# The start of an attention and two-layer network kernel: own banks for x, w_lo in parts, other load order, fewer spins

## The reference

```python
for t in range(S):
    kt, vt, rt, wt = (k[:, :, t], v[:, :, t], r[:, :, t], w[:, :, t])
    cur = np.einsum('bhd,bhe->bhde', u[None] * kt, vt)
    y[:, :, t] = np.einsum('bhd,bhde->bhe', rt, state + cur)
    state = wt[:, :, :, None] * state + np.einsum('bhd,bhe->bhde', kt, vt)
# x = y as [3072, 384]
h = x @ w_in;  g = h * np.clip(h + 3.0, 0.0, 6.0) / 6.0;  x = g @ w_out
h = x @ w_in2; g = h * (1.0 / (1.0 + np.exp(-h)));        x = g @ w_out2
```

## Time and profile before

| | us |
|---|---|
| median of three runs | 890.62 (890.15 to 891.52) |
| profiled execution, its own time | 890.26 |
| span in the profile | 888.6 |
| PE busy | 884.1 (99%) |
| DVE, ACT, POOL busy | 477.6, 314.6, 124.5 |

### The profile page before, as it was taken

How to read it: one execution, slowest core, us unless ns; L and a number is a source line. 1 busy time by engine, 2 the same in 40 slices (tenths; PEclk the granted TensorE clock), 3 DMA queues, 4 the chain that set the end, 5 groups by cost and what they waited for, 6 DMA issues and landing times.

```text
span 888.6 us, 14887 instructions
## 1 busy us (share of the span) xinstructions
PE 884.1 (99%) x5608; PEld 733.8 (83%) x5608; DVE 477.6 (54%) x718; ACT 314.6 (35%) x543; POOL 124.5 (14%) x136
## 2 busy tenths in 40 slices
PE   9999999999999999999999999999999999999998
PEld 7888888888888888888888888888888888888897
DVE  9898667747754864776445443342433343342423
ACT  5634233333233333333444543333232333333222
POOL 2133224304322340342000000000000000000000
PEclk9999999999999999999999999999999999999999
DMA  9545323314422431351223000200200200200201
GB/s 275 174 143 166 92 75 105 93 59 107 126 58 71 126 100 62 93 140 24 107 71 107 1 1 1 36 1 1 35 0 0 35 0 0 35 0 0 36 1 36
DMA packets 89874, 57.61 MB, mean 65 GB/s; under 512 B 76144, under 2 KB 77296, under 8 KB 89840
## 3 DMA queue, kind: packets, MB, share of 16 engines
q1 hardware_dynamic: 89840, 57.15, 23.7%
HBM read 47.18 MB, written 9.96 MB: 64 GB/s over the span
## 4 chain that ended last, share of the span: by engine, by line
PE 98%; DVE 1%; DMA 0%; issue 0%; DVEq 0%
PE bank L882 15%; PE bank L884 15%; PE bank L883 15%; PE bank L906 14%; PE bank L908 13%; PE bank L907 13%; PE bank L937 3%; PE bank L964 2%; PE bank L956 2%; PE bank L945 1%; PE bank L920 1%; PE bank L918 1%; PE bank L919 1%; PE bank L969 1%; PE bank L997 1%; DMA unit_in<-w_fm 0%
## 5 line engine op out<-in xcount | busy, mean ns | idle before, releaser
L882 PE MATMUL bank<-x_hi,w_hi 128*128 (+1 forms) x576 | 226.7, 393 | 0.0
L884 PE MATMUL bank<-x_hi,w_lo 128*128 (+1 forms) x576 | 224.4, 390 | 0.0
L883 PE MATMUL bank<-x_lo,w_hi 128*128 (+1 forms) x576 | 224.3, 389 | 0.0
L494 ACT CAST g_hi<-g 128x512 fp32r<-128x512 f32 x192 | 119.3, 621 | 286.4 <-PE bank L908 221.6
L906 PE MATMUL bank<-g_hi,w_hi 128*128 128x512 f32 x528 | 206.1, 390 | 0.0
L908 PE MATMUL bank<-g_hi,w_lo 128*128 128x512 f32 x528 | 205.5, 389 | 0.0
L907 PE MATMUL bank<-g_lo,w_hi 128*128 128x512 f32 x528 | 205.4, 389 | 0.0
L669 DVE TENSOR_TENSOR g<-g,bank 128x512 f32<-128x512 f32 x96 | 66.0, 687 | 226.0 <-ACT g L488 226.0
L676 DVE TENSOR_TENSOR g_lo<-g,g_hi 128x512 fp32r<-128x512 f32 x192 | 144.9, 755 | 4.4 <-ACT g_hi L494 4.4
L882 PEld LDWEIGHTS bank<-x_hi,w_hi 128*128 128x128 f32 x576 | 108.1, 188 | 24.5 <-issue 0.3
L884 PEld LDWEIGHTS bank<-x_hi,w_lo 128*128 128x128 f32 x576 | 108.1, 188 | 22.8
(11 more groups left out here) (102 smaller groups left out, 653.6 us busy)
## 6 DMA issues: line engine op xcount, KB each, us to landing
unit_in<-rkv_tm SPq DMA_DIRECT2D x20, 576.0 KB, 5.8
unit_in<-rk_fm SPq DMA_DIRECT2D x22, 448.0 KB, 4.6
unit_in<-w SPq DMA_DIRECT2D x9, 768.0 KB, 4.3
x<-w SPq DMA_DIRECT2D x7, 768.0 KB, 7.3
unit_in<-w_fm SPq DMA_DIRECT2D x23, 226.2 KB, 5.4
passing<-tmp SPq DMA_DIRECT2D x20, 256.0 KB, 2.0
keys_tok<-passing SPq DMA_DIRECT2D x80, 64.0 KB, 2.5
out<-tmp SPq DMA_DIRECT2D x60, 64.0 KB, 2.2
```

What stands on the lines that cost most here:

```text
L494: nc.scalar.copy(g_hi[:, p, :], g[:, p, :]).then_inc(ghi_done, 1)
L882: nc.tensor.matmul(h_ps[j % 2][:, :], wh, xh, start=k == 0, stop=False)
L883: nc.tensor.matmul(h_ps[j % 2][:, :], wh, xl, start=False, stop=False)
L884: last = nc.tensor.matmul(h_ps[j % 2][:, :], wl, xh, start=False, stop=k == KT - 1)
```

## The change

- Each x gets a bank of its own (banks 4, 3, 2, 5); `first_values` no longer waits for `xlo`, and starts on the even heads' half of the mask. `xlo` of all four units goes behind the last mask on DVE.
- `first_hidden` replaces `hidden` for tiles 0 and 1: hi*hi (waits for `xhi`), then the low weights (waits for one part of `w_lo`), then the low x.
- `w_lo` of chunks 0 and 1 is made in parts of 1, 1, 2 and 1, 3 tiles.
- The first unit's decays are loaded and scanned in two halves; decays and features of the next unit go ahead of the values of the one before.
- Unit 3's own sums come behind unit 1's values; its keys are turned into bank 7.
- Spins: one fewer after unit 0, and the spins before unit 3's own sums, before unit 2's values and before the first tile go.
- ACT: `first_state(3)` before `whi(1)`; `whi(2)` behind the first tile's `gate` and `ghi`. The memset of `v_mid` moves from DVE to POOL.

```diff
-        first_outer, first_keys, first_x, first_sums = bank[2], bank[3], bank[4], bank[7]
-        last_x = first_scores[0][0]
+        first_sums = bank[7]
+        first_outer = [bank[2], bank[2], bank[2], bank[7]]
+        first_keys = [bank[3], bank[3], bank[3], bank[7]]
+        first_x = [bank[4], bank[3], bank[2], bank[5]]
+        Q0_FIRST, Q0_THEN = (0, 1, 3, 6), (4, 9, 7, 10)
+        Q1_FIRST, Q1_THEN = (2, 5, 8, 11), (1, 4, 7, 10)
...
-            first_load(0)
-            first_load(1)
-            first_load(2)
+            first_decays_load(0)
+            first_features_load(0)
+            first_u_load()
+            first_decays_load(1)
+            first_features_load(1)
+            first_values_load(0)
+            first_decays_load(2)
+            first_features_load(2)
+            first_values_load(1)
+            first_decays_load(3)
+            first_features_load(3)
             load_raw(0)
-            first_load(3)
+            first_values_load(2)
+            first_values_load(3)
             load_raw(1)
...
-            xhi(2, 2, 0, first_x)
-            xhi(3, 3, 0, last_x)
+            xhi(2, 2, 0, first_x[2])
+            xhi(3, 3, 0, first_x[3])
+            first_state(3)
             whi(1)
-            first_state(3)
-            whi(2)
             for j in range(2):
                 tile(j, j, ACT.Relu)
+                if j == 0:
+                    whi(2)
                 if j in WHI_SLOTS:
                     whi(WHI_SLOTS[j])
...
             def scan(a, w, loaded, count):
...
+                    dve.wait_ge(half_loaded, 16)
+                    scan_back(w, HALF, PAIRS * SEG).then_inc(half_scanned, 1)
+                    dve.wait_ge(loaded, count)
+                    scan_back(w, 0, HALF).then_inc(back_done, 1)
...
+            wlo_tiles(0, 0, 1, part_done)
+            for b in range(B):
+                xlo(b, b, 0, first_x[b])
+            wlo_tiles(0, 1, 2, part_done)
+            wlo_tiles(0, 2, 4, wlo_done)
+            wlo_tiles(1, 0, 1, part_done)
             gated(0, 0, 1.0, ALU.min)
+            wlo_tiles(1, 1, 4, wlo_done)
             glo(0, 0)
...
             def first_values(b):
-                if 0 < b < B - 1:
-                    pe.wait_ge(xlo_done, b)
+                v, scores, x_bank = firsts[b][2], a_sets[b % 2], first_x[b]
+                if b == 1:
+                    pe.wait_ge(kt_kept, B - 1)
+                elif b == 2:
+                    pe.wait_ge(added, 2 * (B - 1))
+                pe.wait_ge(v_mid_done, b + 1)
+                pe.wait_ge(masked, 2 * b + 1)
+                for n in Q0_FIRST + Q0_THEN:
...
                 pe.wait_ge(masked, 2 * b + 2)
...
+            def first_hidden(j):
+                pe.wait_ge(whi_done, 1)
+                pe.wait_ge(xhi_done, B)
+                for k in range(KT):
+                    nc.tensor.matmul(h_ps[j][:, :], w_in(w_hi, j, k), x_half(x_hi, 0, k), start=k == 0, stop=False)
+                pe.wait_ge(part_done, j + 1)
...
+                pe.wait_ge(xlo_done, B)
...
-            spin_matmuls(odd, 2)
+            spin_matmuls(odd, 1)
             first_own(1)
...
-            pe.wait_ge(own_done, B - 1)
-            spin_matmuls(first_sums, 1)
+            first_values(1)
             first_own(3)
-            first_values(1)
             spin_matmuls(odd, 2)
             first_turn(3)
             first_raw_scores(3)
-            pe.wait_ge(own_done, B)
-            spin_matmuls(first_sums, 2)
             first_values(2)
             first_values(3)
             first_outer_product(3)
-            spin_matmuls(first_sums, 2)
-            pe.wait_ge(xlo_done, B)
             for j in range(2):
-                hidden(j, j, 0, 0)
+                first_hidden(j)
```

More of the change, by code:

```diff
@@ L408, in _ @@
             nc.gpsimd.memset(half[:, :], 0.5).then_inc(sums_a, 2)
+            nc.gpsimd.memset(v_mid_all, 0.0).then_inc(v_mid_zeroed, 1)
             def first_products(b):
@@ L596, in _ @@
             first_diagonal(1)
-            xhi(0, 0, 0, first_x)
+            xhi(0, 0, 0, first_x[0])
             first_state(1)
@@ L957, in from_state, with from_scores @@
                 last.then_inc(queries_read, 1)
-            def from_scores(b, a, v, scores, x_bank, first):
+            def from_scores(b, a, v, scores, x_bank):
                 pe.wait_ge(v_mid_done, a + 1)
@@ L963, in from_scores @@
                     values = v_mid[b % 2][:, i, 0, :] if e == 1 else v[:, n * Q:n * Q + Q]
-                    last = nc.tensor.matmul(region(x_bank, n), values, scores[:, e // 2 * PAIRS + i, :], start=first and n < 4, stop=False)
-                if first:
-                    last.then_inc(queries_read, 1)
+                    nc.tensor.matmul(region(x_bank, n), values, scores[:, e // 2 * PAIRS + i, :], start=False, stop=False)
                 for n in range(1, REGIONS, 3):
@@ L1024, in first_outer_product @@
                 pe.wait_ge(kt_kept, b + 1)
-                outer(b, kt_tok, KROWS, firsts[b][2], first_outer)
+                outer(b, kt_tok, KROWS, firsts[b][2], first_outer[b])
             def first_values(b):
-                if 0 < b < B - 1:
-                    pe.wait_ge(xlo_done, b)
-                pe.wait_ge(masked, 2 * b + 2)
-                from_scores(b, b, firsts[b][2], a_sets[b % 2], first_x if b < B - 1 else last_x, True)
+                v, scores, x_bank = firsts[b][2], a_sets[b % 2], first_x[b]
[6 more added lines that the diff above has]
+                for n in Q0_FIRST + Q0_THEN:
+                    i, e = n // 3, n % 3
+                    values = v_mid[b % 2][:, i, 0, :] if e == 1 else v[:, n * Q:n * Q + Q]
+                    nc.tensor.matmul(region(x_bank, n), values, scores[:, i, :], start=n in Q0_FIRST, stop=False)
+                pe.wait_ge(masked, 2 * b + 2)
+                for n in Q1_FIRST:
+                    last = nc.tensor.matmul(region(x_bank, n), v[:, n * Q:n * Q + Q], scores[:, PAIRS + n // 3, :], start=False, stop=False)
+                last.then_inc(queries_read, 1)
+                for n in Q1_THEN:
+                    last = nc.tensor.matmul(region(x_bank, n), v_mid[b % 2][:, n // 3, 1, :], scores[:, PAIRS + n // 3, :], start=False, stop=True)
+                last.then_inc(y_full, 1)
+            def first_hidden(j):
[4 more added lines that the diff above has]
+                pe.wait_ge(part_done, j + 1)
+                for k in range(KT):
+                    nc.tensor.matmul(h_ps[j][:, :], w_in(w_lo, j, k), x_half(x_hi, 0, k), start=False, stop=False)
+                pe.wait_ge(xlo_done, B)
+                for k in range(KT):
+                    last = nc.tensor.matmul(h_ps[j][:, :], w_in(w_hi, j, k), x_half(x_lo, 0, k), start=False, stop=k == KT - 1)
+                last.then_inc(hidden_full, 1)
             pe.wait_ge(filled, 1)
```

74 lines of the change are left out of this document (46 added, 28 removed).

## The result

The changed kernel takes 889.07 us (median of 22 runs, 888.49 to 890.17), the kernel before 890.52 in its 22 runs on the same chip. The ratio is 0.9981, 95% interval 0.9974 to 0.9987: a gain of 1.45 us, just inside what was called no change. The prediction was 889.6.

A forecast was written before the change was run, and what follows sets the result against it. PE bounds the kernel, with DVE's queue setting the start of the tiles. First tile 2.70 earlier, a 1.7 wait at `sums(1)` leaving 1.0: span 887.6, median 889.6 us; own range 889.1 to 890.1, 80% range 888.3 to 890.7.

The forecast's parts named there:

- the landing of chunk 3: Load before `whi(3)`: issued 29.39, landed 35.39 after 6.0, so `sums(1)` at 38.94 and PE stands 1.7 us.
- ACT's chain: From first `gate` (29.24) to `whi(3)` at 34.57, 1.63 earlier, not 2.70, as `whi(2)` moved in; `sums(1)` at 38.01.
- rival 1: At `sums(1)`: chunk 3 lands in time, ACT's chain alone decides; gain 1.9, 888.7 us; chance 20%.
- the forecast: Whole kernel: chunk 3's load delays `sums(1)`, leaving 1.0 of 2.70; 889.6 us median; chance 45%.
- The start of the first tile: `first_hidden` on PE starts at 26.85 instead of 29.55, 2.70 us earlier.
- The first scan: DVE's start: decays in two halves, 2.7 us per half load, DVE gains 0.45; `v_mid` memset move worth nothing by itself.
- The two `xlo`: DVE before unit 2's mask: `xlo` of units 0 and 1 leave the path, 0.47 each, 0.94 together.
- The spins: PE before the first tile: the six spins removed only filled waits of PE.
- The load order: Beginning loads: new order costs nothing; tightest is unit 2's v, landed at 18.5, needed at 18.6.
- Rival 2: At `sums(1)`: no new wait at all, the whole 2.7 gained, 887.9 us; chance 8%.
- Rival 3: Before the first tile: beginning hardly moves, a late value load, `xhi` or PE order; gain 0.3, 890.3 us; chance 17%.
- Rival 4: PE's clock: fewer spins and the `sums(1)` hole bring another slow stretch, 1.6 us lost, 891.2 us; chance 10%.

The follow-up runs named there:

- `glo(1)` ahead: Changed kernel with `glo` of tile 1 put ahead of `gated` of tile 2 on DVE; 888.44 us.
- two kernels that share one edit: Changed kernel with `glo(1)` ahead of `gated(2)` on DVE, 888.44 us; the same with unit 0's values also loaded ahead of unit 1's features, 888.37 us.

## Why the prediction was nearly right, step by step

**What held.** PE bounds, DVE's queue sets the start of the tiles, and part of what is won there is given back at `sums(1)`, where `glo(1)` is late. The trace shows this wait, `glo(1)` ahead takes it away, and by that the time falls further.

**The step that was mis-sized is the landing of chunk 3.** I took 6.0 us from the one row of that load, and so let the load decide: PE standing 1.7. It landed in 4.4, and in 4.2 to 4.6 in all twelve experiments, the one on the kernel before included (4.6). Then ACT's chain decides, as rival 1 had it: `whi(3)` at 34.80 against its 34.57, `sums(1)` at 38.24 against its 38.01. Both are 0.23 off as the first `gate` started at 29.47, not 29.24; the 3.44 from `whi(3)` to PE came out to the hundredth. PE stood 0.80. The one row that I took was a slow one. More rows alone would not have told: the page of before has the loads of that size in two groups, the median of one is 7.3, and that of all 16 is the same 6.0. Eight of the nine in the other group, though, were issued from 423 us on with little else in the queue (the ninth, at 16.13, took 7.4), and they were the better price:

```profile
unit_in<-w SPq DMA_DIRECT2D x9, 768.0 KB, 4.3
x<-w SPq DMA_DIRECT2D x7, 768.0 KB, 7.3
```

So in the trace this is rival 1, not the forecast. For the profiled execution rival 1 gives 890.26 - 1.9 = 888.36 and the forecast 889.26; measured was 888.64. For the median they give 888.7 and 889.6, and 889.07 lies between, just under the forecast's own range of 889.1 to 890.1. One reason is that the start of the first tile varies from execution to execution: 27.12 in one trace and 28.00 in another of the same kernel.

**The start of the first tile.** 2.70 predicted, 2.43 in the one trace and 1.55 in the other. Its parts:

- *The first scan*: 0.45 predicted, 5.35 - 4.61 = 0.74 in the trace. But the split itself is worth 0.24 there, as the kernel with whole decays shows; the rest is that the whole load landed in 2.6 in that kernel and not in 3.1 (3.0 in the kernel before with six spins fewer), and that DVE's memsets end at 3.2, not at 3.7, so that it can use this. I had called the moved memset worth nothing, which holds only beside the slow landing. The Trainium skill, "DMA: Bandwidth & Descriptors", section "Anatomy of one DMA", gave an estimate of 2.27 for a half and 2.53 for the whole; measured were 2.1 and 2.2, and for the whole 2.6 once and 3.0 and 3.1 in the two traces with the old kernel's beginning. So it was nearer than my 2.7 for the half; for the whole the traces lie on both sides.
- *The two `xlo`*: 0.94 predicted on DVE's path, 0.6 to 0.8 measured in time. Right, or a little high.
- *The masks of units 2 and 3*: predicted 22.98 and 24.38, measured 22.89 and 24.35, with the wait between them. Right in this trace; in the second trace of the same kernel they stand at 23.77 and 25.23, so that they came out to a tenth is luck. From there 26.85 became 27.12, as PE's outer product and `xhi(3)` (26.49) came 0.2 later.
- *The spins*: I wrote that they only filled waits. That failed: put back, they cost 2.3 to 2.5, 1.85 of it in the span. Each had stood beside a wait that the other parts make shorter; in the kernel before, taking them out alone gives 0.87, 0.5 of it in the span.
- *The load order*: I wrote that it costs nothing, and looked only for loads that come late. That it gains 1.3 to 1.6 I missed. I never asked what POOL does when the features come late, nor what DVE does beside POOL.

The parts don't add up. Undone one by one they give between 2.3 + 1.3 + 0.6 + 0.1 = 4.3 and 2.5 + 1.6 + 0.8 + 0.3 = 5.2, and the change as a whole is worth 1.5: they hold up the same path, and either the spins or the load order, left as before, gives the whole gain away. The banks of their own, `first_hidden` with `w_lo` in parts, and the later own sums of unit 3 were not undone alone, so what each is worth isn't known.

That the sum came near is in part luck. It followed the chain of starts in one trace, and two errors of opposite sign meet in it: the wait at `sums(1)` was put at 1.7 and was 0.80, and the first tile was put at 26.85 and started at 27.12, and at 28.00 in the second trace of the same kernel. The two terms put at nothing, the spins and the load order, are among the largest.

**Where the gain of the changed `whi(2)` went.** I wrote that ACT's chain gained 1.63 rather than 2.70 because `whi(2)` was moved into it. The kernel with `whi(2)` back shows the same chain (7.85 from the first tile to `whi(3)` against 7.68). The arithmetic to 34.57 was right but for the 0.23 above; the reason was wrong.

**The rivals.** Rival 2 (no wait at all) fell: the wait is there. Rival 3 (the beginning hardly moves) fell. Rival 4, the clock, did not come true in the changed kernel's traces, with 1.00 granted in every stage, but it is real: five more spins gone bring it, and so can one late load (last section).

**What stays open.** Why the warm-up's 18 rows last 5.97, 6.68 or 7.39 in different executions, though the profile shows no difference ahead of them, wasn't settled. The 0.9 between the two traces' first tiles is not due to it: there ACT's copy waited for the load of the values until 10.84, 0.89 later than in the first trace, and the first tile is 0.88 later. Why the six spins lengthen the time around the span is open as well. Whether 888.4 is truly below 889.1 rests on two kernels that share one edit, 0.6 to 0.9 below the changed one, and on the wait that their traces lack.

## What to carry to other kernels

Price a wait on a load from the rows of its size that found the queue equally idle, with their spread, not from the one row of that load nor from all rows together (both gave 6.0 here): 6.0 against 4.4 decided which of two chains was the later. Compare two traces at an early point that the edit can't have moved before reading a later one: here 0.5 us was there before the edit came into play. When a change shortens a stage, go again through everything that filled its waits (spins above all): what was free in a long wait is on the path in a short one. And where a small operation of another engine gets its data later, look at what runs beside it, not only at who waits for it.

## What the runs showed of the hardware

**A DVE scan stands while POOL multiplies.** Both read from SBUF. The scan takes 1.21 alone. Overlap is POOL's end minus DVE's start; the lines are, in this order, from the changed kernel, the kernel before, the old load order (two), and the kernel before with six spins fewer:

| POOL's operation | DVE's scan starts | overlap | scan takes | over 1.21 |
|---|---|---|---|---|
| 17.93 to 19.21 | 18.92 | 0.29 | 1.39 | 0.18 |
| 13.44 to 14.73 | 14.40 | 0.33 | 1.41 | 0.20 |
| 13.89 to 15.17 | 14.34 | 0.83 | 1.92 | 0.71 |
| 19.26 to 20.54 | 20.08 | 0.46 | 1.55 | 0.34 |
| 19.66 to 20.94 | 20.46 | 0.48 | 1.57 | 0.36 |

The excess is the overlap less about 0.12, whatever its length: DVE doesn't run at half speed but waits until POOL is done. The Trainium skill, "SBUF — State Buffer", section "Who interferes with whom", says that a DVE instruction with two SBUF inputs contends with a GpSimd instruction that reads SBUF. These rows agree, and so do those of the other traces (overlaps of 0.2 to 0.9). That the shared ports are an exclusive lock, as the same section of the Trainium skill calls them, fits the other way round too: POOL stands while DVE works. Its product below began 0.52 before DVE's `glo(0)` was over and took 1.40; in the kernel before the same product, with DVE idle, took 1.01.

```profile
32.07 0.69 DVE L706 TENSOR_TENSOR g_lo<-g,g_hi 128x512 fp32r<-128x512 f32 x1
32.24 1.40 POOL L458 TENSOR_TENSOR unit_in<-unit_in 128x384 f32<-128x384 f32 x1 [8.01 <-DVE w_lo L715]
```

**A load's landing varies from execution to execution.** Chunk 3 took 6.0 in one trace and 4.2 to 4.6 in the thirteen others. Unit 0's values, issued at 4.12, took 5.8 in one trace of the changed kernel and 6.7 in the other, and 8.0 in that of the kernel with two `xlo` back.

**The clock fell after short waits of PE.** In the kernel without spins, waits of a few tenths and one of 0.95 were followed by two stretches at half clock, one of them over 6 us long; in the median of the twelve runs that kernel is 1.3 us slower than the changed one. The same happens with no spin missing. In the profiled execution of the kernel with two `xlo` back PE waited 1.46 for unit 0's values, the granted clock was 0.50 from 14 to 26, and the first tile started at 35.05:

```profile
12.16 0.57 PE L994 MATMUL bank<-unit_in,keys_tok 128*48 128x48 f32 x16 [1.46 <-DMA unit_in<-rkv_tm]
```

Nor does every wait do it. In the kernel with `glo(1)` ahead and unit 0's values first PE was busy 1.17 of the 2 us from 10 to 12, and in the kernel before with six spins fewer 1.39 and 1.29 in the two stretches from 26 to 30, and in both the granted clock stayed at 1.00. Which wait brings the clock down these runs don't tell.
